# Second layer's first product by Strassen's scheme: seven block products, in three tiles of 768 tokens

## The chip, the cores and the metric

One program runs on one core of a Trainium2 chip. A core has TensorE (PE, matrix products, with its weight loads shown as PEld), VectorE (DVE), ScalarE (ACT), GpSimd (POOL) and SyncE (SP, which here only starts transfers). Each works through its own list of instructions in order, and they wait for each other by semaphores. The metric is the device time of one execution in microseconds (us); lower is better.

## The reference, cut to what matters

```
attn_out = softmax attention over means of 4 tokens, repeated 4 times
           + softmax attention within +-3 tokens          # 4 x 8 heads x 576 tokens x 64
x = attn_out as [2304, 512]
h = x @ w_in;   x = (s * relu(h)**2 + b) @ w_out          # 512 -> 2048 -> 512, first layer
h = x @ w_in2;  g = h - tanh(h);  out = g @ w_out2        # 512 -> 2048 -> 512, second layer
```

All values are float32. The change is in the last line alone.

## The kernel before, in words

**Numbers in two parts.** TensorE is fed with the type fp32r. Each operand a is kept as a "high" part (ACT copies a into an fp32r tile) and a "low" part (DVE or POOL subtracts the high part from a). A product is three matmuls that add up in PSUM: high by high, low by high, high by low.

**Stages.** Attention comes first, on all engines. The first layer runs over eight tiles of 288 tokens, and beside it runs the attention of the tokens to come. Its result goes turned, channels first, through the DRAM tensor x2T (ystage to x2T, `store1`), and the second layer loads it from there (`load_x2`).

**Second layer.** Six tiles of 384 tokens (`N2 = 384`, `TILES2 = 6`). Each tile has 16 turns f, one for 128 of the 2048 inner channels. A turn is:

- `hidden2` (L1922 to L1939): 12 matmuls (4 parts of the 512 channels, 3 products of parts), 384 columns each, into one of the two PSUM banks of `hid`.
- `tanh` (ACT, L1638), `difference` (DVE, `gdif`, L1361), `g2_high` (ACT, L1646), `g2_low` (DVE, L1370), one after the other, on 128 x 384 values.
- `output2` (L1941 to L1957), three turns later: 9 matmuls of 512 columns (3 groups of 128 tokens, 3 products of parts) that add into three banks of `acc` over the whole tile. In the last tile the last two turns of it are `last2` (L1967).

**Weights and tokens of the second layer.** The two weight matrices are loaded 1 MB at a time during the last tile of the first layer into the places of the first layer's weights (L938, L950) as soon as these are used up, and split once, 512 columns per instruction (`w2_high` on ACT, L1621, `w2_low` on DVE, L1343). They stay for all six tiles. The tokens of a tile are loaded (`load_x2`, L965) and split (`x2_split_high` on ACT, L1630, `x2_split_low` on DVE, L1351) a tile ahead, in two buffers. POOL has no work in the second layer.

**Order.** `plan()` lists all steps with an estimated cost, what they come after, and a rank; `Plan.run` places them one by one, the one that can start earliest first and the lower rank among equals, and so writes the order of each engine's list. The order is fixed when the program is built. It knows no interruption of an instruction and no effect of one engine on another's speed.

**First layer, where it touches the change.** POOL makes the low part of each turn's activations (`g_low`, `gl`, L1057, 128 x 288) between ACT's work and the `output1` of three turns later.

Of the kernel before, what the change touches and what calls it, by code (L numbers as in the profile page):

```python
# [49 lines left out]
N2 = 384  # L50
TILES2 = TOKENS // N2
LAG2, GRING2 = 3, 4
# [43 lines left out]
def turn_of(f, half):  # L96

    return f + LAG1 * half

# [131 lines left out]
def plan():  # L231
# [189 lines left out]
    for kind, turn in turns(TILES1, LAG1):  # L421
# [30 lines left out]
    for g in range(FT // WGROUP):  # L452
        for kind, user in (("load_w2a", "hidden1"), ("load_w2b", "output1")):
            o.add("SP", 0.6, (3, g), (kind, g), [(user, last, WGROUP * (g + 1) - 1)], kbytes=1024)
    for f in range(FT):
        for half in range(2):
            o.add("ACT", act(512), (2, f), ("w2_high", f, half), [(("load_w2a", "load_w2b")[half], f // WGROUP)])
            o.add("DVE", dve(512), (2, f), ("w2_low", f, half), [("w2_high", f, half)])
    for j in range(TILES2):
        after = [("x2_split_low", j - 1)] if j else [("add_up", SUBS - 1, NPART - 1)]  # L460
        o.add("SP", 0.6, (3, j), ("load_x2", j), after + [("store1", last_tile(j))], kbytes=800)
        o.add("ACT", KT * act(N2), (0,), ("x2_split_high", j),
              [("load_x2", j)] + ([("hidden2", j - 2, FT - 1)] if j > 1 else []))
        o.add("DVE", KT * dve(N2), (0,), ("x2_split_low", j), [("x2_split_high", j)])
    for kind, turn in turns(TILES2, LAG2):
        j, f = divmod(turn, FT)
        if kind == "hidden":
            after = [chain] + ([("w2_low", f, 0)] if j == 0 else [])
            after += [("x2_split_low", j)] if f == 0 else []
            after += [("difference", *divmod(turn - 2, FT))] if turn > 1 else []  # L470
            o.add("PE", 12 * mm(N2), (1,), ("hidden2", j, f), after)
            chain = ("hidden2", j, f)
            o.add("ACT", act(N2), (0,), ("tanh", j, f),
                  [chain] + ([("difference", *divmod(turn - 2, FT))] if turn > 1 else []))
            o.add("DVE", dve(N2), (0,), ("difference", j, f), [("tanh", j, f)])
            o.add("ACT", act(N2), (0,), ("g2_high", j, f), [("difference", j, f)] + (
                [("output2", *divmod(turn - GRING2, FT))] if turn >= GRING2 else []))
            o.add("DVE", dve(N2), (0,), ("g2_low", j, f), [("g2_high", j, f)])
        else:
            after = [chain, ("g2_low", j, f)] + ([("w2_low", f, 1)] if j == 0 else [])  # L480
            if f == 0:
                after += [("finish2", j - 1, i) for i in range(N2 // P)] if j else [("finish1", last)]
            if j == TILES2 - 1 and f >= FT - 2:

                if f == FT - 1:
                    for i in range(N2 // P):
                        o.add("PE", 6 * mm(DM), (1,), ("last2", i), after + [("g2_low", j, f - 1)])
                        after = [("last2", i)]
                    for i in range(2):
                        o.add(("DVE", "ACT")[i], 0.7, (0,), ("finish2", j, i), [("last2", i)])  # L490
                        o.add("SP", 1.2, (0, j, i), ("store_out", j, i), [("finish2", j, i)], kbytes=256)
                    for e in ("DVE", "ACT"):
                        o.add(e, 0.7, (0,), ("finish_last", e), [("last2", 2)])
                    o.add("SP", 0.6, (0, j, 2), ("store_out", j, 2), [("finish_last", "DVE")], kbytes=128)
                continue
            o.add("PE", 9 * mm(DM), (1,), ("output2", j, f), after)
            chain = ("output2", j, f)
            if f == FT - 1:
                for i in range(N2 // P):
                    o.add(("DVE", "ACT", "DVE")[i], 0.7, (0,), ("finish2", j, i), [chain])  # L500
                    if i != 1:
                        o.add("SP", 1.2, (0, j, i), ("store_out", j, i), [("finish2", j, i)], kbytes=256)
# [17 lines left out]
def build(nc, q, k, v, moe_w_in, moe_w_out, moe_s, moe_b, moe2_w_in, moe2_w_out, out):  # L520
# [104 lines left out]
    at[0] = o_att  # L625
    x2h, _ = place("x2h", [P, 2, KT, N2], F32R)
    x2l, _ = place("x2l", [P, 2, KT, N2], F32R)
    x2raw, _ = place("x2raw", [P, KT, N2], F32)
    tanh, _ = place("tanh", [P, 2, N2], F32)
    gdif, _ = place("gdif", [P, 2, N2], F32)  # L630
    ostage, _ = place("ostage", [P, 3, DM], F32)

    g2h, _ = place("g2h", [P, GRING2, N2], F32R, o_x)
    g2l, _ = place("g2l", [P, GRING2, N2], F32R, o_xh)
    assert GRING2 * N2 <= XRING * KT * NS
# [17 lines left out]
    s_x2raw = sem("s_x2raw")  # L653

# [12 lines left out]
    s_w2high, s_w2low = sem("s_w2high"), sem("s_w2low")  # L667
# [14 lines left out]
    s_x2h, s_x2l, s_h2, s_tanh = sem("s_x2h"), sem("s_x2l"), sem("s_h2"), sem("s_tanh")  # L682
    s_dif, s_g2h, s_g2l, s_used2 = sem("s_dif"), sem("s_g2h"), sem("s_g2l"), sem("s_used2")
    s_o = [sem(f"s_o{i}") for i in range(3)]
    s_last, s_oh = sem("s_last"), sem("s_oh")
    s_out = [sem(f"s_out{i}") for i in range(3)]
# [77 lines left out]
    def half_of(f, half, a, b):  # L764
        return a[:, :, f * P:(f + 1) * P] if half == 0 else b[:, f, :]
# [63 lines left out]

    def rows_of(j, i):  # L830
# [13 lines left out]
    def stored_count(j, i):  # L844

        return sum(len(rows_of(one, i)) for one in range(j + 1))

    def store_rows(e, j, i):
        for rows, row, pattern in rows_of(j, i):
            e.dma_start(dram(out, row * DM, pattern), ostage[rows, i, :]).then_inc(s_out[i], 16)  # L850

    def store_half(e, half):

        rows, row, pattern = rows_of(TILES2 - 1, 2)[half]
        e.dma_start(dram(out, row * DM, pattern), ostage[rows, 2, :]).then_inc(s_out[2], 16)
# [206 lines left out]
    def vector_program(ve):  # L1062
# [9 lines left out]
        for kind, *key in o.order["DVE"]:  # L1072
# [929 lines left out]
```

## Time and profile before

| | us |
|---|---|
| median of 3 runs | 911.38 |
| lowest and highest run | 910.88, 911.38 |
| span of the profiled execution | 909.3 |
| PE busy in it | 895.9 (99%) |
| DVE, ACT, POOL busy | 501.7, 425.0, 279.4 |
| chain that ended last: PE, ACT, DMA, DVE | 95%, 2%, 1%, 1% |

The span reaches from the first to the last instruction of the profiled execution. The profiled execution is given by its span alone; the median of the runs is 2.1 us above it, which is what lies around the span. The page's 40 slices of 22.7 us show PE at 9 tenths or more from the second to the 39th. The granted TensorE clock shows 9 (90% or more) in all of them, and its mean over the span is 0.998. From the 24th slice on DVE and ACT are busy two or three tenths, and POOL not at all: that is the second layer. A matmul's busy time is more than the time until the next one starts, since matmuls overlap; the time between starts is read from the chain or the timeline.

### The profile page before, as it was taken

Reading aid. Unit: us, or ns where it says so; the run is one execution under the profiler, and the core shown is the slowest. Engines: PE = TensorE matmul, PEld = TensorE weight load, DVE = VectorE, ACT = ScalarE, POOL = GpSimd, SP = SyncE. Lnnn points to the kernel's source line nnn. Section 1 sums busy time; section 2 is a strip of 40 time slices with the busy share of each in tenths; the row PEclk is TensorE's granted clock in tenths of the full one; section 3 lists DMA queues with packets and bytes.
Section 4 is the critical chain, followed back from the end, with each engine's and each line's share of the span. In section 5 each row is a group of like instructions: output and inputs, shape, how many; then the busy total and the mean of one; then the engine's idle time right before and its main releaser. Section 6 shows DMA issues by size and latency. Waiting matters only on the chain.

```text
span 909.3 us, 15682 instructions
## 1 busy us (share of the span) xinstructions
PE 895.9 (99%) x6100; PEld 846.0 (93%) x6100; DVE 501.7 (55%) x635; ACT 425.0 (47%) x1060; POOL 279.4 (31%) x280
## 2 busy tenths in 40 slices
PE   6999999999999999999999999999999999999998
PEld 6789999999999999999999999999999999999997
DVE  5658599989999999982104632323323323322322
ACT  2899585566546754446457722322323223222221
POOL 6568474966497653534222000000000000000000
PEclk9999999999999999999999999999999999999999
DMA  8962453343344223002225400200200100100101
GB/s 217 274 236 55 127 146 85 91 121 85 97 114 115 62 61 78 19 2 65 66 77 181 165 1 1 70 1 1 70 1 22 49 1 1 35 1 1 35 1 35
DMA packets 48333, 65.15 MB, mean 72 GB/s; under 512 B 18246, under 2 KB 30084, under 8 KB 48260
## 3 DMA queue, kind: packets, MB, share of 16 engines
q1 hardware_dynamic: 45865, 62.42, 24.8%
q10 hardware_dynamic: 2395, 1.74, 0.8%
q8 instruction: 48, 0.79, 0.4%
q14 instruction: 25, 0.20, 0.1%
HBM read 54.71 MB, written 9.44 MB: 71 GB/s over the span
## 4 chain that ended last, share of the span: by engine, by line
PE 95%; ACT 2%; DMA 1%; DVE 1%; issue 1%; SPq 1%; ACTq 0%; DVEq 0%
PE acc L1918 22%; PE hid L1937 22%; PE hid L1890 21%; PE acc L1955 21%; PE pa L1848 1%; PE pa L1815 1%; DMA dkey<-in_k_dram 1%; PE pa L1832 1%; PE pa L1690 1%; PE pa L1861 1%; PE acc L1967 0%; PE hid L1898 0%; SPq L867 0%; PE hid L1796 0%; PE pa L1753 0%
## 5 line engine op out<-in xcount | busy, mean ns | idle before, releaser
L1057 POOL TENSOR_TENSOR gl<-relu,gh 128x288 fp32r<-128x288 f32 x128 | 128.6, 1008 | 185.9 <-PE acc L1918 129.5
L1361 DVE TENSOR_TENSOR gdif<-hid,tanh 128x384 f32<-128x384 f32 x96 | 53.5, 558 | 184.4 <-ACT tanh L1638 184.2
L1918 PE MATMUL acc<-gh,wbh 128*128 128x288 f32 (+1 forms) x512 | 154.6, 302 | 0.0
L1890 PE MATMUL hid<-xh,wah 128*128 128x288 f32 x512 | 153.5, 301 | 0.3 <-ACT relu L1597 0.2
L1918 PE MATMUL acc<-gl,wbh 128*128 128x288 f32 (+1 forms) x512 | 151.5, 296 | 0.0
L1918 PE MATMUL acc<-gh,wbl 128*128 128x288 f32 (+1 forms) x512 | 151.1, 295 | 0.0
L1890 PE MATMUL hid<-xh,wal 128*128 128x288 f32 x512 | 150.4, 295 | 0.0
L1890 PE MATMUL hid<-xl,wah 128*128 128x288 f32 x484 | 142.0, 294 | 0.0
L1638 ACT ACTIVATE tanh<-hid 128x384 f32<-128x384 f32 x96 | 47.2, 491 | 186.3 <-PE hid L1937 186.3
L1937 PE MATMUL hid<-x2h,wal 128*128 128x384 f32 x384 | 129.0, 336 | 0.0
L1937 PE MATMUL hid<-x2h,wah 128*128 128x384 f32 x384 | 128.9, 336 | 0.0
L1937 PE MATMUL hid<-x2l,wah 128*128 128x384 f32 x384 | 128.8, 336 | 0.0
L1597 ACT ACTIVATE relu<-hid 128x288 f32<-128x288 f32 x128 | 52.3, 409 | 134.0 <-PE hid L1890 110.7
L1955 PE MATMUL acc<-wbl,g2h 128*128 128x512 f32 x282 | 110.2, 391 | 0.0
L1955 PE MATMUL acc<-wbh,g2l 128*128 128x512 f32 x282 | 110.0, 390 | 0.0
L1955 PE MATMUL acc<-wbh,g2h 128*128 128x512 f32 x282 | 109.9, 390 | 0.0
L1918 PEld LDWEIGHTS acc<-gh,wbh 128*128 128x128 f32 x512 | 96.5, 189 | 1.0 <-issue 0.4
L1890 PEld LDWEIGHTS hid<-xh,wah 128*128 128x128 f32 x512 | 96.2, 188 | 1.0 <-issue 0.6
L1918 PEld LDWEIGHTS acc<-gh,wbl 128*128 128x128 f32 x512 | 96.5, 188 | 0.0
L1918 PEld LDWEIGHTS acc<-gl,wbh 128*128 128x128 f32 x512 | 96.4, 188 | 0.0
L1890 PEld LDWEIGHTS hid<-xh,wal 128*128 128x128 f32 x512 | 96.3, 188 | 0.1
L1890 PEld LDWEIGHTS hid<-xl,wah 128*128 128x128 f32 x484 | 90.8, 188 | 0.0
(162 smaller groups left out, 1549.9 us busy)
## 6 DMA issues: line engine op xcount, KB each, us to landing
wa_raw<-in_moe_w_in_dram SPq DMA_DIRECT2D x8, 1024.0 KB, 7.8
wb_raw<-in_moe_w_out_dram SPq DMA_DIRECT2D x8, 1024.0 KB, 6.3
kl<-in_k_dram SPq DMA_DIRECT2D x23, 240.0 KB
vl<-in_v_dram SPq DMA_DIRECT2D x23, 240.0 KB
x2T<-ystage SPq DMA_DIRECT2D x8, 576.0 KB, 3.2
x2raw<-x2T SPq DMA_DIRECT2D x6, 768.0 KB, 4.5
own<-in_q_dram SPq DMA_DIRECT2D x11, 384.0 KB
ql<-in_q_dram SPq DMA_DIRECT2D x24, 144.0 KB, 2.9
```

The source lines that it names most:

```text
L1057: g.tensor_tensor(out=gl[:, turn % LRING1, 0:NS], in0=relu[:, f % 2, :], in1=gh[:, turn % GRING1, 0:NS].bitcast(F32), op=ALU.subtract).the ...
L1361: ve.tensor_tensor(gdif[:, f % 2, :], hid[:, f % 2, 0:N2], tanh[:, f % 2, :], ALU.subtract).then_inc(s_dif, 1)
L1597: sc.activation(r, hid[:, f % 2, 0:n], ACT.Relu).then_inc(s_relu, 1)
L1638: sc.activation(tanh[:, f % 2, :], hid[:, f % 2, 0:N2], ACT.Tanh).then_inc(s_tanh, 1)
L1690: one = pe.transpose(pa[0:HD, r, g * P:(g + 1) * P], src[:, g0 + g, :], ident[:, :])
L1815: one = pe.matmul(pa[0:2 * TQ, r, x * GROUPS:(x + 1) * GROUPS], apart[:, hp, x, :, :].rearrange("p t n -> p (t n)"), plain[:, hp, :], star ...
L1832: one = pe.transpose(pa[0:HG, r, x * 2 * TQ:(x + 1) * 2 * TQ], pc[0:2 * TQ, ones.start + x, kh * HG:(kh + 1) * HG], ident[0:2 * TQ, 0:2 * TQ])
L1848: one = pe.matmul(pa[h2 * HD:(h2 + 1) * HD, r, 0:cols.stop - cols.start], vd[0:HG, kh, 2 * hp + h2, :], pT[0:HG, h2, kh, cols], start=kh = ...
L1890: one = pe.matmul(dst, w[:, d, cols], x[:, j % XRING, d, :], start=i == 0, stop=i == 3 * KT - 1)
L1918: one = pe.matmul(acc[:, d, n], w[:, f, cols], g[:, turn % ring, n], start=(f == 0 and p == 0), stop=(f == FT - 1 and p == 2))
L1937: one = pe.matmul(hid[:, f % 2, 0:N2], w[:, d, f * P:(f + 1) * P], x[:, j % 2, d, :], start=(d == 0 and p == 0), stop=(d == KT - 1 and p = ...
L1955: one = pe.matmul(acc[:, i, :], g[:, f % GRING2, i * P:(i + 1) * P], w[:, f, :], start=(f == 0 and p == 0), stop=(f == FT - 1 and p == 2))
```

## The change

The first product of the second layer (x @ w_in2) is no longer 16 turns of 12 matmuls per tile. The token tile becomes 768 wide, three tiles. The 512 input channels are halved (A/B index 1 and 2), the 768 tokens of a tile are halved, and the inner channels are taken in pairs of 128. For each such pair ("quad" q, 8 per tile, block n = 8j + q) the 2 x 2 by 2 x 2 block product is made with seven products in place of eight (Winograd's form of Strassen's scheme). A product has 6 matmuls of 384 columns: two parts of 128 channels (kk) and the three products of parts.

```
S1 = A21+A22, S2 = S1-A11, S3 = A11-A21, S4 = A12-S2        (weights)
T1 = B12-B11, T3 = B22-B12, T2 = T3+B11, T4 = B21-T2        (tokens)
```

What is new in each place:

- PE, per block: `p1 p6 out p2 p7 out p4 p5 out p3 out out out`, where the six `out2` are those of the block before (6 matmuls of 512 columns each, six groups of 128 tokens, in four banks of `acc` and two of `pa`). All seven products share the two banks of `hid`: p1 then p2 on top of it and later p5, p3 on top of it, in bank 0; p6, then p7, p4 on top of it, in bank 1. Between them DVE and ACT take values out: p2 waits for `copy1` (ACT copies p1), p7 for `u2`, p4 for `u3`, p5 for the first difference, p3 for `c22`, the next p1 for `c12`.
- DVE, per block: five sums with a PSUM operand (u2, u3, c21, c22, c12), four differences, four `g2_low`, all 128 x 384. ACT, per block: `copy1`, four `tanh`, four `g2_high`.
- Weights of the first product: for each of the 8 quads four loads of 128 KB, four sums on DVE (`w2_sums`, 256 columns), one high part on ACT and one low part on POOL, each over 7 x 2 x 128 = 1792 columns in one instruction. Quads 0 and 1 can be loaded after turn 7 of the last tile of layer one, 2 and 3 after its last hidden turn, 4 to 7 after its last output. They stay for all three tiles.
- Weights of the second product no longer stay: for each of the 24 blocks 512 KB are loaded into a ring of two (`load_w2b`) and split by two ACT and two POOL instructions of 512 columns.
- Tokens: per tile seven blocks for each of two kk. POOL makes the four sums T1, T3, T2, T4 and the low parts of T3 and T4, ACT all high parts, DVE the other low parts. There is one buffer in place of two: a block's high part waits for the tile's last product that uses it (`XORDER` follows the order of the products).
- Block 0 takes the last three `output1` of the first layer as its only `out`.
- Results leave through three stages of 512 columns, of which two also hold T1 of the next tile.

```diff
-N2 = 384
+N2 = 768
 TILES2 = TOKENS // N2
-LAG2, GRING2 = 3, 4
+HALF2 = N2 // 2
+QUADS = FT // 2
+BLOCK2 = N2 // P
+PRODUCTS = {"p1": (A11, B11, 0, True), "p6": (S2, T2, 1, True), "p2": (A12, B21, 0, False),
+            "p7": (S3, T3, 1, True), "p4": (A22, T4, 1, False), "p5": (S1, T1, 0, True), "p3": (S4, B22, 0, False)}
+XORDER = (B11, T2, B21, T3, T4, T1, B22)
+POOL_LOWS = (T3, T4)
...
+        order = ["p1", "p6", outs[0], "p2", "p7", outs[1], "p4", "p5", outs[2], "p3"] + outs[3:]
...
+            elif kind == "w2a_low":
+                q, = key
+                g.wait_ge(s_w2ah, q + 1)
+                g.tensor_tensor(out=wql[q][:, :, :, :], in0=wq_raw[q][:, :, :, :], in1=wqh[q][:, :, :, :].bitcast(F32),
+                                op=ALU.subtract).then_inc(s_w2al, 1)
...
+            elif kind == "w2_sums":
+                q, = key
+                raw, a21 = wq_raw[q], wq_a21[q][:, :, :]
+                ve.wait_ge((s_wa + s_wb)[q], 16 + 64)
+                ve.tensor_tensor(raw[:, S1, :, :], a21, raw[:, A22, :, :], ALU.add).then_inc(s_w2sum, 1)
+                ve.tensor_tensor(raw[:, S3, :, :], raw[:, A11, :, :], a21, ALU.subtract).then_inc(s_w2sum, 1)
...
+            elif kind == "u3":
+                n, = key
+                if n:
+                    ve.wait_ge(s_g2l, 4 * (n - 1) + 3)
+                ve.wait_ge(s_u2, n + 1)
+                ve.wait_ge(s_product["p7"], n + 1)
+                ve.tensor_tensor(sum22[:, :], hid[:, 1, 0:HALF2], sum12[n % 2][:, :], ALU.add).then_inc(s_u3, 1)
...
+            elif kind == "product":
+                n, name = key
+                j, q = divmod(n, QUADS)
+                w, x, r, fresh = PRODUCTS[name]
+                if j == 0:
+                    pe.wait_ge(s_w2al, q + 1)
+                if q == 0:
+                    for kk in range(2):
+                        wait_low2(pe, j, kk, x)
...
+                for kk in range(2):
+                    for p, (wt, xt) in enumerate(((wqh[q], x2h), (wqh[q], x2l), (wql[q], x2h))):
+                        one = pe.matmul(hid[:, r, 0:HALF2], wt[:, w, kk, :], xt[:, x, kk, :],
+                                        start=fresh and kk == 0 and p == 0, stop=kk == 1 and p == 2,
+                                        skip_group_check=not fresh)
+                one.then_inc(s_product[name], 1)
...
+            elif kind == "out2":
+                n, i = key
+                j, q = divmod(n, QUADS)
+                if n == 0:
                     pe.wait_ge(s_y, KT * TILES1)
+                elif q == 0:
+                    pe.wait_ge(s_o[i], j)
+                pe.wait_ge(s_w2bl, 2 * (n + 1))
+                pe.wait_ge(s_g2l, 4 * n + (2 if i < BLOCK2 // 2 else 4))
```

## Rows read from the trace of the kernel before

**Rows 1.** The page: span, and busy us (share) xinstructions of each engine.
```profile
span 909.3 us, 15682 instructions
PE 895.9 (99%) x6100; PEld 846.0 (93%) x6100; DVE 501.7 (55%) x635; ACT 425.0 (47%) x1060; POOL 279.4 (31%) x280
```

**Rows 2.** Windows: length, busy us (xcount) of PE, PEld, DVE, ACT, POOL; clock, DMA, GB/s.
```profile
500.00:520.00 20.00, 20.00 (x130) 19.64 (x129) 11.44 (x21) 15.04 (x32) 1.61 (x2) 1.00 0.54 188
600.00:700.00 100.00, 100.00 (x509) 91.16 (x508) 30.39 (x55) 27.82 (x56) 0.00 (x0) 1.00 0.06 17
```

**Rows 3.** The chain of waits: start us, length us, what ran.
```profile
502.30 6.35 PE acc L1918 x48
508.65 8.32 PE hid L1937 x48
...
574.83 4.09 PE acc L1955 x18
578.92 4.16 PE hid L1937 x24
...
901.26 4.09 PE acc L1967 x18
...
905.44 0.68 DVE ostage L1386
```

**Rows 4.** Groups by shape: operation, tiles, shapes xcount | busy us, mean ns | idle before.
```profile
L1937 PE MATMUL hid<-x2h,wal 128*128 128x384 f32 x384 | 129.0, 336 | 0.0
L1638 ACT ACTIVATE tanh<-hid 128x384 f32<-128x384 f32 x96 | 47.2, 491 | 186.3 <-PE hid L1937 186.3
L1361 DVE TENSOR_TENSOR gdif<-hid,tanh 128x384 f32<-128x384 f32 x96 | 53.5, 558 | 184.4 <-ACT tanh L1638 184.2
L1646 ACT ACTIVATE g2h<-gdif 128x384 fp32r<-128x384 f32 x96 | 50.4, 525 | 67.9 <-DVE gdif L1361 67.9
L1351 DVE TENSOR_TENSOR x2l<-x2raw,x2h 128x384 fp32r<-128x384 f32 x24 | 12.7, 590 | 25.1 <-ACT x2h L1630 25.1
L1621 ACT ACTIVATE wah<-wa_raw 128x512 fp32r<-128x512 f32 x16 | 9.9, 619 | 0.0
```

**Rows 5.** Timeline near the end: start us, us, engine, line, operation [idle before <-releaser].
```profile
892.87 0.39 PE L1955 MATMUL acc<-wbh,g2h 128*128 128x512 f32 x1
893.13 0.49 ACT L1638 ACTIVATE tanh<-hid 128x384 f32<-128x384 f32 x1 [2.33 <-PE hid L1937]
893.75 0.56 DVE L1361 TENSOR_TENSOR gdif<-hid,tanh 128x384 f32<-128x384 f32 x1 [2.30 <-ACT tanh L1638]
894.40 0.53 ACT L1646 ACTIVATE g2h<-gdif 128x384 fp32r<-128x384 f32 x1 [0.78 <-DVE gdif L1361]
```

**Rows 6.** Timeline in the attention: POOL, DVE, and a PE step that waits for DVE.
```profile
32.57 1.28 POOL L1040 TENSOR_TENSOR wal<-wa_raw,wah 128x512 fp32r<-128x512 f32 x1
32.82 1.39 DVE L1110 TENSOR_TENSOR dprob<-dprob,dinv 128x330 f32<-128x330 f32 x1
34.26 0.25 PEld L1780 LDWEIGHTS acc<-ident,dprob 128*66 128x66 f32 x3 [0.83 <-DVE dprob L1110]
```

**Rows 7.** Timelines of POOL and DVE side by side, at three places.
```profile
77.06 1.55 POOL L1040 TENSOR_TENSOR wal<-wa_raw,wah 128x512 fp32r<-128x512 f32 x1
77.39 1.78 DVE L1178 TENSOR_TENSOR wal<-wa_raw,wah 128x512 fp32r<-128x512 f32 x1
...
157.55 3.27 POOL L1031 TENSOR_TENSOR own<-own 128x384 f32<-128x384 f32 x1
159.86 1.17 DVE L1336 TENSOR_TENSOR xraw<-pa,up 128x256 f32<-128x256 f32 x2
...
497.60 0.82 POOL L1057 TENSOR_TENSOR gl<-relu,gh 128x288 fp32r<-128x288 f32 x1 [2.38 <-PE acc L1918]
498.00 0.96 DVE L1343 TENSOR_TENSOR wal<-wa_raw,wah 128x512 fp32r<-128x512 f32 x1 [1.03 <-ACT wah L1621]
498.89 0.68 DVE L1343 TENSOR_TENSOR wbl<-wb_raw,wbh 128x512 fp32r<-128x512 f32 x1
```

**Rows 8.** Transfers: tiles, queue xcount, KB each, median us to landing.
```profile
x2T<-ystage SPq DMA_DIRECT2D x8, 576.0 KB, 3.2
wa_raw<-in_moe_w_in_dram SPq DMA_DIRECT2D x8, 1024.0 KB, 7.8
```

More of the change, by code:

```diff
@@ L420, in plan @@
                 o.add("POOL", 1.15, (0,), ("x_low", j, d), [("x_high", j, d)])
-    for kind, turn in turns(TILES1, LAG1):
+    for kind, turn in turns(TILES1, LAG1)[:-LAG1]:
         j, f = divmod(turn, FT)
@@ L451, in plan @@
     last = TILES1 - 1
[L452 to L458, printed above, removed]
-    for j in range(TILES2):
[L460 to L491, printed above, removed]
-                    for e in ("DVE", "ACT"):
[L493 to L502, printed above, removed]
@@ new lines, in plan @@
+    for q in range(QUADS):
+        after = [("hidden1", last, 7)] if q < 2 else [("hidden1", last, FT - 1)] if q < 4 else [("output1", last, FT - 1)]
+        if q == QUADS - 1:
+            after.append(("store1", last))
+        o.add("SP", 2.4, (3, 2 * q), ("load_w2a", q), after, kbytes=512)
+        o.add("DVE", 1.8, (2, q), ("w2_sums", q), [("load_w2a", q)])
+        o.add("ACT", 1.65, (2, q), ("w2a_high", q), [("w2_sums", q)])
+        o.add("POOL", 4.7, (2, q), ("w2a_low", q), [("w2a_high", q)])
@@ L622, in build @@
     lpT = behind("lpT", [P, BLOCKS, P], *room_band)
[L625 to L635, printed above, removed]
+    unit, quad = 4 * HALF2, 4 * 2 * 7 * 2 * P
@@ new lines, in build @@
+    o_ring = o_wbh
+    o_quads = [o_wah, o_wal, o_wah + quad, o_wal + quad] + [o_ring + 4 * 8 * DM + quad * i for i in range(3)]
+    o_g2 = o_x
+    o_quads.append(o_g2 + 4 * 4 * 4 * HALF2 * 2 // 2)
+    o_x2 = o_quads[-1] + quad
+    o_inter = o_x2 + 4 * 2 * 7 * 2 * HALF2
+    o_raw0 = o_inter + 5 * unit
+    o_raw1 = o_quads[6] + quad
+    assert o_raw1 + 4 * unit <= o_x and o_raw0 + 4 * unit <= nc.sbuf_usable_end and o_x2 >= o_att
+    wqh = [place(f"wqh{i}", [P, 7, 2, P], F32R, o_quads[i])[0] for i in range(QUADS)]
@@ new lines, in build @@
+    tanh11, _ = place("tanh11", [P, HALF2], F32, o_inter + 3 * unit)
+    tanh, _ = place("tanh", [P, HALF2], F32, o_inter + 4 * unit)
+    odd12, _ = place("odd12", [P, HALF2], F32, o_wal + 2 * quad + 4 * DM)
+    sum12 = (even12, odd12)
+    ostage = [place(f"ostage{i}", [P, DM], F32, o)[0]
+              for i, o in enumerate((o_wah + 2 * quad, o_wah + 2 * quad + 4 * DM, o_wal + 2 * quad))]
+    assert o_wal + 2 * quad + 4 * DM + unit <= o_wbh and o_wah + 2 * quad + 8 * DM <= o_wal
+    raw0, _ = place("x2raw0", [P, 2, N2], F32, o_raw0)
@@ L1889, in tensor_program @@
                             pe.wait_ge(s_x0l, d + 1)
-                    one = pe.matmul(dst, w[:, d, cols], x[:, j % XRING, d, :], start=i == 0, stop=i == 3 * KT - 1)
+                    one = pe.matmul(dst, w[:, group, d, cols], x[:, j % XRING, d, :], start=i == 0, stop=i == 3 * KT - 1)
                 if f or not j:
```

540 lines of the change are left out of this document (382 added, 158 removed).

## The prediction

> **What bounds the kernel now.** The page comes first: PE is busy 895.9 of 909.3 us, no other engine over 55% [rows 1]. A busy share says nothing yet of who is waited for, so the windows by stage are next: in the second layer PE is busy without a gap, 100.00 of 100.00 us, at full granted clock, DVE 30.4, ACT 27.8, POOL 0.0 [rows 2]. The chain of waits then shows that the end hangs on PE: from 508.65 us on, over the whole listing, `hidden2` and `output2` alternate with nothing between, to `last2` at 901.26, and only the last eviction follows, at 905.44 [rows 3]. From the chain come the times per matmul, too: 24 of `hidden2` in 4.16 us and 48 in 8.32, so 0.1733 us each; 18 of `output2` in 4.09, so 0.227 each. (The mean of 336 ns in the groups [rows 4] is the time in flight, not the pitch.) 1152 x 0.1733 + 864 x 0.227 = 199.7 + 196.1 = 395.8 us, and the chain has 905.35 - 508.65 = 396.7. The second layer is as long as its matmuls. So fewer matmuls pay in full, as long as the other engines, now less than a third busy, keep up.
>
> **What is removed.** Per tile of 768 and pair of 128 channels, the old form takes 2 x 4 x 3 matmuls for each half of the tokens, 48; seven products of six are 42. Over 24 blocks that is 1008 for 1152, all of the same 384 columns: 144 x 0.1733 = **-25.0 us**. `output2` keeps its 24 x 36 = 864. I take no price for changing groups more often: between the last `hidden2` matmul and the next step PE goes on at its pitch, though the new group has waits of its own [rows 5]. Bounds: 0 to 0.05 us (the time from a DVE end to PE's weight load, below) for each of the 312 groups less the 192 before, at most 6 us.
>
> **A block without disturbance.** A product takes 6 x 0.1733 = 1.04 us, an `out` 6 x 0.227 = 1.36, a block 7 x 1.04 + 6 x 1.36 = 15.45. Latencies from rows: PE to ACT 0.26 after the start of the next group (892.87 to 893.13), ACT to DVE 0.13, DVE to ACT 0.09 [rows 5], DVE to PE 0.05 (32.82 + 1.39 = 34.21 to 34.26) [rows 6]. The tightest waits are p4 on `u3` and p3 on `c22`, each with one `out` as its cover: 0.26 + 0.56 + 0.05 = 0.87 of 1.36, so DVE may be 0.49 late, some 0.27 if the weight load is to keep its lead of one matmul. Before `u3` stands the first difference: p2's end + 0.26 + 0.49 + 0.13 = 0.88, then 0.56, so DVE is free at 1.44, when `u3` could have begun at 1.04 + 0.26 = 1.30. It is 0.14 late, within the slack. p2 and p7 have cover of 2.4, the next p1 of 4.1. DVE's 13 operations of 0.56 are 7.3 us of 15.45, ACT's nine of 0.5 and two of 0.62 are 5.7. So an undisturbed block costs nothing. I take 1.5 us for all of them (bounds 0 and 24 x 2 x 0.3 = 14, if every such wait is 0.3 late). The tail is as before, six matmuls per group and halves at the end: 0.
>
> **The seam between the layers.** Block 0 has only three `out`. So p3 is followed at once by the next p1, which waits for c12: 0.26 + 0.56 + 0.05 = 0.87, and a weight load of 0.2: **+1.1 us**. Bounds 0.9 and 4 (if `finish1` on ACT is late too).
>
> **What POOL's new work does to DVE.** This is the large unknown. In the second layer POOL was idle; now it has 8 instructions of 1792 columns (`w2a_low`), 48 of 512 and 36 of 384. Its durations alone: 0.82 for 288 columns, 1.28 for 512 [rows 6, 7], 2.05 ns per column more, so 1.02 for 384 and **3.9 us for 1792**. The rows show what such an instruction does to DVE. POOL runs 77.06 to 78.61; a DVE subtraction of 512 columns with both operands in SBUF begins at 77.39 and takes 1.78, where it takes 0.68 alone (498.89): it ends 0.56 after POOL, as if it had stood still until then. Likewise 0.96 at 498.00 under a POOL instruction that ends at 498.42. But at 159.86 two DVE sums with one operand in PSUM take 1.17 together, inside a POOL instruction of 3.27 [rows 7]. So the five sums and the first difference of a block are free of it, and seven operations of a block (three differences, four `g2_low`), the 32 weight sums and the low parts of the tokens can each be held up for as long as one POOL instruction. DVE's list is in order, so `u3` and `c22` behind a held one are late as well.
>
> Only blocks of tile 0 meet the long ones. Quads 0 and 1 are made under the first layer, where a turn takes 24 x 0.132 = 3.2 us (6.35 us for 48 matmuls [rows 3]), POOL works 0.82 of it, and `output1` wants its result three turns, 9.5 us, after `hidden1`. One long instruction in front of it is covered: 0, or 2 x 1 us if two meet. Quads 2 to 7 come while blocks 0 to 3 run: 6 x 3.9 = 23 us of POOL. I place one such instruction at any point of a block. In the first four us after the block's last `g2_low` it holds nothing up; before the first `g2_low` it makes c22 up to 2.0 late (mean 0.5); later it makes c12 or the next u2 up to 2.3 late (mean 0.3 to 1.4). The mean over the block is 0.5 us. Where the four sums of the next quad (256 columns, 0.44 each by 0.56 for 384 and 0.68 for 512) are held in front of `u3` or `c22`, the lateness is up to 3.9 + 1.7 - 0.3, and its mean some 2.5. The quads' loads come close together, so I count four of the six at 2.0 and two at 0.5: **+9 us**. ACT's high part of 1792 columns (0.525 for 384 and 0.619 for 512 [rows 4], so 1.6) can make a `tanh` late too; that lies within these. Bounds: 0 (every one falls in a free place) and 23 (each is added in full).
>
> The Trainium skill says the same more sharply than the rows, which show no POOL instruction of 3.9 us without contention: "SBUF — State Buffer", section "Who interferes with whom", has a DVE instruction with two SBUF inputs and a GpSimd one that reads SBUF exclude each other, the first one holding the ports for its whole instruction. By it the upper bound of 23 us is possible; if a long instruction gave way between, the term would be near 1.
>
> **Changes of tile.** Twice, DVE gets 10 low parts of 0.59, ACT 14 high parts and half of six evictions, POOL some eight sums and low parts of 1.02 that hold DVE as above. They have two blocks (30.9 us) from the last p1 of a tile. DVE then has 2 x 7.3 + 5.9 + 2.0 = 22.5 us of work and perhaps 4 of holding, so no bound by throughput, but an operation of 0.6 in front of `u3` or `c22`, or one POOL instruction of 1.02, exceeds the 0.27 to 0.49. Ten such meetings of 0.25 us: **+5 us** for both. Bounds 0 and 16 x 1.02 = 16.
>
> Transfers: 512 KB per block against a median of 3.2 us for 576 KB [rows 8]. Landing 3.3 us after the block's start, ACT 1.2 and POOL 2.6 later, they are ready at 7.1, and wanted 17.5 us after that start. 0, with POOL's work beside them. These POOL instructions of 1.28 fall between 4 and 7 us of a block, mostly before its first `g2_low` at 6.6.
>
> **The sum.** -25.0 + 1.1 + 9 + 5 + 1.5 = -8.4. Made against the profiled span of 909.3 it gives 900.9; with the 2.1 us that the median of 911.38 lies above that span, **903 us**.
>
> **Rivals.**
> *Everything stays covered.* For it: DVE less than half busy, waits with slack in an undisturbed block, the order's own ranks. Against it: the held DVE operations of rows 7. -25.0 + 1.1 + 0.5: 888 us. Chance 0.22.
> *POOL and DVE exclude each other so much that it is slower.* Place: blocks 0 to 3. In about 60 us POOL's 23 + 10 (four blocks of `w2b_low`) + 4 (token sums) and DVE's 28 x 0.56 + 24 x 0.44 = 26 want the same thing, 63 us in all. Then PE waits nearly as long as POOL's long instructions last. It decides from the point where the held time exceeds the saved 25. -25.0 + 1.1 + 23 + 10 (tile changes at twice my term) + 2 = +11: 922 us. Against it: POOL and DVE also wait for loads and for ACT, which leaves gaps, and PE has 1.4 to 4 us of cover at most points. Chance 0.2.
> *The short covers fail in every block.* p4 and p3 each 0.3 late: 48 x 0.3 = 14.4, on top of 1.1 and 5, with the weights at 1: -3.5, 908 us. Against it the 0.49 worked out above. Chance 0.08.
> *The likeliest*, chance 0.5: 895 to 911.
>
> **How the numbers follow.** A measurement of this kernel tells 0.2%, 1.8 us, from no change. Faster: all of the first rival, 0.45 of the likeliest, 0.05 of the third, 0.72 together. Slower: the second rival, 0.20. Within 0.2%: the rest, 0.08. The range is to hold 8 in 10: from the covered case, 889 with a little loss, to 916, inside the slower case.
>
> **What would show it.** 42 matmuls on PE per block at 0.173, and a clean block of 15.45 us. PE's idle time should be put down to DVE, at p4 (u3), p3 (c22) and p1 (c12), and lie in the first four blocks and around the two changes of tile. There DVE operations with two SBUF operands should last 1 to 4.5 us in place of 0.56, each beginning under a POOL instruction, while u3 and c22 stay at 0.56. `w2a_low` should take 3.9 us. I am wrong if the clean blocks are longer than 15.6 us, if the pitch rises above 0.174, if the first layer's last tile gets longer, or if DVE is not held by the long instructions.

## The result, and the profile after

| | before | after |
|---|---|---|
| median of nine runs, us | 911.19 | 913.32 |
| lowest and highest | 909.78, 912.35 | 911.63, 914.59 |
| ratio, 95% interval | | 1.0028 [1.0018, 1.0038] |
| span of the profiled execution, us | 909.3 | 909.8 |
| its own time, us | | 912.1 |
| mean granted clock in it | 0.998 | 0.990 |

The prediction was 903 us, 8.4 faster; the kernel became 2.1 us slower. (913.3 lies within the stated 889 to 916, but on the other side of 911.) The saved matmuls are really gone, yet the time is not. First the page of the changed kernel, which answers to [rows 1]: the span, the engines' busy time, and two rows of the 40 slices.

```profile
span 909.8 us, 15887 instructions
PE 881.7 (97%) x5956; PEld 825.6 (91%) x5956; DVE 586.3 (64%) x759; ACT 465.6 (51%) x1128; POOL 421.9 (46%) x372
PE   6999999999999999999999787999999999999998
...
PEclk9999999999999999999999989999999999999999
```

There are 144 matmuls fewer (5956 for 6100), and PE is busy 14.2 us less, at a span 0.5 longer. The slices say where to look: PE falls from 9 to 7 and 8 in the 23rd to 25th, just where the second layer begins, and the granted clock falls with it in the 24th. The windows, which answer to [rows 2] (length, busy us of PE, PEld, DVE, ACT, POOL, clock, DMA, GB/s), give the size:

```profile
500.00:520.00 20.00, 15.32 (x99) 14.58 (x97) 13.35 (x17) 7.62 (x12) 14.20 (x8) 0.99 0.28 80
520.00:545.00 25.00, 20.29 (x79) 17.82 (x80) 20.10 (x28) 10.30 (x15) 10.77 (x5) 0.80 0.39 118
545.00:572.00 27.00, 21.82 (x101) 19.06 (x102) 17.86 (x23) 9.86 (x19) 10.50 (x4) 0.94 0.12 39
600.00:700.00 100.00, 99.55 (x497) 88.96 (x496) 54.79 (x93) 43.40 (x87) 32.63 (x26) 1.00 0.23 69
```

From 600 on PE is nearly as dense as before. Between 500 and 572 it stands idle 4.7 + 4.7 + 5.2 = 14.6 us, and the clock means 0.80 and 0.94. The chain of waits, which answers to [rows 3], shows a block without disturbance (start, length, what ran):

```profile
567.83 2.10 PE hid L2234 x12
569.93 1.39 PE acc L2251 x6
571.32 2.08 PE hid L2234 x12
573.40 1.39 PE acc L2251 x6
...
580.70 2.73 PE pa L2251 x12
583.43 2.10 PE hid L2234 x12
```

Twelve matmuls, of two products, in 2.08 are 0.1733 each, as before, and from 567.83 to 583.43 a block takes 15.60; over all matmul starts it is 15.61. Laying those starts out by block gives the account ("clean" is a block without disturbance, "over clean" what a block took beyond it):

```
block      0      1      2      3-6    7      8      9-14   15     16     17-22
took       18.08  24.27  22.77  15.61  15.75  16.61  15.61  15.71  16.57  15.61
over clean  5.98   8.66   7.16  0      0.14   1.00   0      0.10   0.96   0
(clean: 12.10 for block 0, whose only outs are the three output1 of 1.59 each; 15.61 for the others)
```

The last three `output1` of the first layer stand in block 0 now. With them counted in, the stretch to the end of the last matmul was 401.4 us before and is 403.2 now. Who holds PE up in the first three blocks is in the waits of PE (us in total, times, longest), from 502 to the end:

```profile
PE hid L2234 <- DVE sum L1613: 5.8, 3, 3.1
PE hid L2234 <- DVE even L1619: 4.1, 1, 4.1
PE acc L2251 <- DVE g2l L1633: 3.4, 1, 3.4
PE hid L2234 <- DVE odd L1619: 0.9, 1, 0.9
...
```

L1613 is `c22`, ahead of p3; L1619 is `c12`, ahead of the next p1; L1633 is `g2_low`, ahead of an `out2`. All three are DVE; the rest of the list is 1.1 us. But these are not slow operations themselves. Two timelines side by side, POOL first, then DVE (start, us, operation, idle before):

```profile
510.13 8.32 POOL L1241 TENSOR_TENSOR wql<-wq_raw,wqh 128x1792 fp32r<-128x1792 f32 x2 [2.89 <-ACT wqh L1883]
530.33 4.17 POOL L1241 TENSOR_TENSOR wql<-wq_raw,wqh 128x1792 fp32r<-128x1792 f32 x1 [11.89 <-ACT wqh L1883]
537.39 4.15 POOL L1241 TENSOR_TENSOR wql<-wq_raw,wqh 128x1792 fp32r<-128x1792 f32 x1 [2.88 <-ACT wqh L1883]
...
544.79 4.16 POOL L1241 TENSOR_TENSOR wql<-wq_raw,wqh 128x1792 fp32r<-128x1792 f32 x1 [0.93 <-ACT wqh L1883]
```

```profile
512.26 2.34 DVE L1633 TENSOR_TENSOR g2l<-tanh,g2h 128x384 fp32r<-128x384 f32 x1
514.52 0.55 DVE L1613 TENSOR_TENSOR sum<-hid,sum 128x384 f32<-128x384 f32 x1
514.99 3.87 DVE L1628 TENSOR_TENSOR sum<-sum,tanh 128x384 f32<-128x384 f32 x1
...
530.52 4.26 DVE L1574 TENSOR_TENSOR wq_raw<-wq_raw,wq_a 128x256 f32<-128x256 f32 x1
...
537.57 4.25 DVE L1576 TENSOR_TENSOR wq_raw<-wq_raw 128x256 f32<-128x256 f32 x1
...
545.00 4.23 DVE L1574 TENSOR_TENSOR wq_raw<-wq_raw,wq_a 128x256 f32<-128x256 f32 x1
```

Read the starts and ends together. The two POOL instructions of 510.13 end at about 514.3 and 518.45; the `g2_low` of 512.26 ends at 514.60, the difference of 514.99 at 518.86. A weight sum of 256 columns that begins 0.2 us after POOL (530.52 after 530.33) takes 4.26 in place of 0.42. The operation at 514.52 in between, `c22`, has an operand in PSUM and takes 0.55 beneath the second POOL instruction. The groups by shape say it for the whole layer (xcount, then busy us and mean ns):

```profile
L1628 DVE TENSOR_TENSOR sum<-sum,tanh 128x384 f32<-128x384 f32 x48 | 32.6, 680 | 1.5 <-ACT tanh L1922 1.5
L1633 DVE TENSOR_TENSOR g2l<-tanh,g2h 128x384 fp32r<-128x384 f32 x24 | 18.7, 781 | 11.5 <-ACT g2h L1929 11.5
L1613 DVE TENSOR_TENSOR sum<-hid,sum 128x384 f32<-128x384 f32 x24 | 13.3, 555 | 7.7 <-PE hid L2234 7.7
L1574 DVE TENSOR_TENSOR wq_raw<-wq_raw,wq_a 128x256 f32<-128x256 f32 x6 | 11.3, 1876 | 0.0
```

Same size, both operands in SBUF: 680 and 781 ns in the mean. One in PSUM: 555. The last row is the costliest: 1876 ns for an operation of 420. The held operations explain the waits in two ways. In block 0 it is a difference of the block itself, held at 514.99, that makes `c12` late, and PE waits 4.1 us. In block 2 a `g2_low` held at 557.62 (3.72 us, under POOL's instruction of 556.88) makes `c22` late by 1.8. And in blocks 1 and 2 the DVE list places the four sums of a later quad in front of `c22`, `c12` or a `g2_low` of the running block, POOL holds one of them for four us (530.52, 537.57, 545.00), and what PE waits for stands behind it, by 3.1, 0.9 and 3.4 us.

The second toll is TensorE's clock. The timeline of PE around 520, matmuls of the same shape (the one at 515.63 is from before the wait):

```profile
515.63 0.34 PE L2234 MATMUL hid<-x2h,wql 128*128 128x384 f32 x1
...
520.62 0.66 PE L2234 MATMUL hid<-x2h,wqh 128*128 128x384 f32 x1 [4.11 <-DVE even L1619]
521.08 0.52 PE L2234 MATMUL hid<-x2l,wqh 128*128 128x384 f32 x1
521.40 0.52 PE L2234 MATMUL hid<-x2h,wql 128*128 128x384 f32 x1
```

After 4.11 us of idling the pitch is 0.32 in place of 0.173. The granted clock stands at half, 1.2 GHz, from 519.69 for 6.83 us, from 536.76 for 3.41 and from 550.41 for 3.41. Each of these begins in the last microsecond of a wait of PE of 3.1 to 4.1 us. Windows laid inside the three stretches (13.4 us in all) show PE busy for 12.0, so up to half of that, 6 us, is the clock's toll (an estimate).

### The profile page after: what moved, and what is told of

Read it like the earlier page. It is cut to its first block, busy times and chain, and to the rows that moved or that the text cites. A ratio compares the mean times of both kernels' runs of the same rounds, so it can differ in the third digit from the quotient of the medians.

```text
span 909.8 us, 15887 instructions
## 1 busy us (share of the span) xinstructions
PE 881.7 (97%) x5956; PEld 825.6 (91%) x5956; DVE 586.3 (64%) x759; ACT 465.6 (51%) x1128; POOL 421.9 (46%) x372
## 4 chain that ended last, share of the span: by engine, by line
PE 88%; DVE 7%; ACT 2%; issue 2%; DMA 1%; SPq 1%; ACTq 0%; DVEq 0%
PE acc L2197 22%; PE hid L2169 21%; PE hid L2234 18%; PE acc L2251 13%; PE pa L2251 6%; DVE wq_raw L1574 1%; PE pa L2127 1%; PE pa L2094 1%; DVE sum L1628 1%; DMA dkey<-in_k_dram 1%; PE pa L2111 1%; PE pa L1969 1%; DVE x2l L1583 1%; DVE g2l L1633 1%; PE pa L2140 1%
## 5 line engine op out<-in xcount | busy, mean ns | idle before, releaser
L1233 POOL TENSOR_TENSOR gl<-relu,gh 128x288 fp32r<-128x288 f32 x128 | 131.4, 1031 | 150.1 <-PE acc L2197 106.6
L1249 POOL TENSOR_TENSOR w2bl<-w2b_raw,w2bh 128x512 fp32r<-128x512 f32 x48 | 63.3, 1339 | 211.1 <-ACT w2bh L1890 211.1
L2234 PE MATMUL hid<-x2h,wqh 128*128 128x384 f32 x336 | 115.0, 342 | 12.0 <-DVE sum L1613 5.8
L2234 PE MATMUL hid<-x2l,wqh 128*128 128x384 f32 x336 | 114.0, 339 | 0.0
L2234 PE MATMUL hid<-x2h,wql 128*128 128x384 f32 x336 | 113.7, 338 | 0.0
L2234 PEld LDWEIGHTS hid<-x2h,wqh 128*128 128x128 f32 x336 | 64.0, 190 | 19.9 <-issue 13.6
L2251 PE MATMUL acc<-w2bh,g2h 128*128 128x512 f32 x192 | 75.9, 396 | 3.4 <-DVE g2l L1633 3.4
L2251 PE MATMUL acc<-w2bh,g2l 128*128 128x512 f32 x192 | 77.0, 401 | 0.0
L2251 PE MATMUL acc<-w2bl,g2h 128*128 128x512 f32 x192 | 76.8, 400 | 0.0
```

Of the source, the lines that this page charges most:

```text
L1233: g.tensor_tensor(out=gl[:, turn % LRING1, 0:NS], in0=relu[:, f % 2, :], in1=gh[:, turn % GRING1, 0:NS].bitcast(F32), op=ALU.subtract).the ...
L1249: g.tensor_tensor(out=w2bl[:, slot, :], in0=w2b_raw[:, slot, :], in1=w2bh[:, slot, :].bitcast(F32), op=ALU.subtract).then_inc(s_w2bl, 1)
L2234: one = pe.matmul(hid[:, r, 0:HALF2], wt[:, w, kk, :], xt[:, x, kk, :], start=fresh and kk == 0 and p == 0, stop=kk == 1 and p == 2, skip_ ...
L2251: one = pe.matmul(out_bank(i), g[:, n % 2, f, i * P:(i + 1) * P], w[:, slot, :], start=(q == 0 and f == 0 and p == 0), stop=(q == QUADS - ...
```

## The experiments

Two theories at the start. A: a POOL instruction holds a DVE operation with two SBUF operands until it ends, so the length of `w2a_low` is what costs. B: the DVE list itself is the fault, four weight sums in one step ahead of what PE waits for. The medians of before beside these runs were 911.19 (first four), 911.22 (next four) and 910.88 (last two); each ratio is against these. In experiments 1, 2, 5 and 6 the time came out 0.2 to 2.3 us below what A had foretold, in 3 it came out 0.8 above.

**1. `w2a_low` in seven instructions of 256 columns**, order and data as they were; PE's wait counts seven pieces per quad.

```diff
-                g.tensor_tensor(out=wql[q][:, :, :, :], ...)
+                for one in range(7):
+                    g.tensor_tensor(out=wql[q][:, one, :, :], ...)
```

> The changed kernel with one edit: POOL makes the low part of a quad's weights in seven instructions of 256 columns instead of one of 1792; order of every list unchanged. Theory A (a POOL instruction shuts out DVE operations with two SBUF operands for its whole length; six long ones cost the new kernel most of the 22 us that blocks 0 to 2 take beyond 12.1, 15.6 and 15.6): no DVE operation is held longer than some 0.8 us, the three blocks take 8 to 12 us beyond the clean length instead of 22, the clock falls less often, time 900 to 904. Theory B (the order is at fault: weight sums stand in DVE's list ahead of u2 and u3; the holding is incidental): the same 1792 columns on POOL, same order, so within 2 us of the changed kernel, 911 to 914.

Measured: 897.74 us, ratio 0.9852 [0.9837, 0.9867]. Blocks 0 to 2 took 14.17, 17.24 and 18.51. The timeline, POOL first and then DVE:

```profile
525.81 12.67 POOL L1242 TENSOR_TENSOR wql<-wq_raw,wqh 128x256 fp32r<-128x256 f32 x14 [3.22 <-ACT wqh L1884]
```

```profile
530.52 0.96 DVE L1577 TENSOR_TENSOR wq_raw<-wq_raw 128x256 f32<-128x256 f32 x1
531.51 0.85 DVE L1579 TENSOR_TENSOR wq_raw<-wq_raw 128x256 f32<-128x256 f32 x1
532.28 1.09 DVE L1629 TENSOR_TENSOR sum<-sum,tanh 128x384 f32<-128x384 f32 x1
533.30 0.55 DVE L1620 TENSOR_TENSOR odd<-hid,odd 128x384 f32<-128x384 f32 x1
```

POOL works longer now, 12.67 for two quads where two whole instructions took 8.32, and DVE is held at every turn, but for one piece each, 0.5 us and not 4. The longest wait of PE was 1.3, and the clock did not fall in this layer. 15.6 us for a cut in one instruction: A holds. POOL's longer work is now itself waited for:

```profile
PE hid L2235 <- POOL wql L1242: 2.4, 3, 1.3
```

**2. The whole `w2a_low`, but later**: those of quads 2 to 7 wait, in the plan and on POOL, for the last `g2_low` of the block two before.

```diff
+                if q > 1:
+                    g.wait_ge(s_g2l, 4 * (q - 2) + 4)
                 g.wait_ge(s_w2ah, q + 1)
```

> The changed kernel with the 1792-column instructions of quads 2 to 7 kept whole but each made to wait for the last g2_low of the block two before the one that uses it, so that one falls in each of blocks 1 to 6 at its start, where DVE has no operation with two SBUF operands for some 6 us. Theory A (place of the long POOL instructions): holds of 4 us vanish or fall where nothing waits; the loss over clean blocks falls from 22 us to 5 to 8, time 896 to 901. Theory B (weight sums ahead of u2, u3 in DVE's list; they are untouched here): loss stays at 12 or more, time 903 to 912. A third view, that the preparation work is simply too much for the engines: no change, 911 to 914.

Measured: 895.70, ratio 0.9824 [0.9808, 0.9841]. Blocks 13.57, 19.76, 15.63, then 15.61. The instructions are as long as ever; spread over the blocks and put where DVE has little of that kind they cost nothing, but for one in block 1 (POOL, then DVE):

```profile
522.67 4.07 POOL L1243 TENSOR_TENSOR wql<-wq_raw,wqh 128x1792 fp32r<-128x1792 f32 x1 [14.81 <-DVE g2l L1635]
```

```profile
523.60 3.42 DVE L1575 TENSOR_TENSOR wq_raw<-wq_a,wq_raw 128x256 f32<-128x256 f32 x1
```

That one made p3 2.3 us late, and the clock fell for 3.41 us behind it. The place counts as much as the length.

**3. The four weight sums as four steps of the plan**, so that urgent work can go between.

```diff
-        o.add("DVE", 1.8, (2, q), ("w2_sums", q), [("load_w2a", q)])
+        for m in range(4):
+            o.add("DVE", 0.43, (2, q), ("w2_sums", q, m), [("load_w2a", q)])
```

> The changed kernel with one edit: the four weight sums of a quad are four steps of the plan instead of one of 1.8 us, so that product steps of the same moment come between; POOL's 1792-column instructions unchanged. Theory A (holding by POOL): at most 3 us gained, 909 to 913, and DVE operations of 4 us still there. Theory B (order): most of the 22 us gained, 895 to 901.

Measured: 913.79, ratio 1.003 [1.002, 1.004], no better than the change itself. Blocks 19.26, 17.68, 29.07, with 20.48 us at half clock. The timeline, POOL and then DVE, shows why the finer order doesn't help: whichever operation with two SBUF operands comes next is caught.

```profile
540.72 4.13 POOL L1242 TENSOR_TENSOR wql<-wq_raw,wqh 128x1792 fp32r<-128x1792 f32 x1 [3.43 <-ACT wqh L1890]
```

```profile
540.89 4.25 DVE L1580 TENSOR_TENSOR wq_raw<-wq_raw 128x256 f32<-128x256 f32 x1
```

B as the main cause falls. What the order costs can be read from block 0: 13.56 with the sums in one step (experiments 2 and 5), 13.04 with the sums apart (6 to 10), so 0.5 us.

**4. What the clock costs.** Twenty matmuls into a bank not in use fill the first long wait, ahead of p1 of block 1; they compute nothing that is used.

```diff
+                    if n == 1:
+                        for _ in range(20):
+                            pe.matmul(pa[:, 1, 0:HALF2], wqh[0][:, 0, 0, :], x2h[:, 0, 0, :], start=True, stop=True)
```

> The changed kernel with 20 more matmuls of 384 columns (3.5 us, results unused) in front of the p1 of block 1, where PE stood idle 4.4 us and after which its granted clock was 0.5 for 6.83 us. Theory C (the idle time takes a second toll through the clock, some 3 us here): block 1 runs its first groups at 1.04 and 1.39 instead of 2.06, 1.92 and 2.27, the first stretch at 0.5 is gone, and the kernel gains 2 to 4 us, 909 to 911. If the clock fell for another reason or the slow groups hid behind DVE anyway: no change or up to 1 us slower, 913 to 914.

Measured: 909.91, ratio 0.9990 [0.9981, 0.9999], 3.4 us below the change. The first stretch at half clock is gone (the next begins at 536.43), the first product of block 1 takes 1.16 for 2.06, and the block 21.59 for 24.27, 2.7 us less. The other two stretches stay. The toll is real; it is a part of what the waits cost, not a cause beside them.

**5. The most that `w2a_low` can cost.** Of quads 2 to 7 only 256 of the 1792 low columns are made, and PE multiplies by the low parts of quads 0 and 1.

```diff
+                some = slice(0, 7) if q < 2 else slice(0, 1)
...
-    ..., (wql[q], x2h))):
+    ..., (wql[q % 2], x2h))):
```

> The changed kernel without the long POOL work: of quads 2 to 7 only 256 of the 1792 columns of the low part are made, and TensorE reads the low parts of quads 0 and 1 in their place; same order of all lists, the eight-in-a-row weight sums and all ACT work kept. Theory A with its price: what is left beyond clean blocks (12.1 for block 0, 15.6 each for 1 and 2) is the seam of 1.1 us and the order's share, 3 to 5 us together, against 22 in the changed kernel and some 7 with seven short instructions: 893 to 897. Theory B (order) would leave 12 us or more: 904 or above.

Measured: 892.82, ratio 0.9800 [0.9784, 0.9815]. Blocks 13.56, 15.75, 15.80, then 15.61. So the long instructions of these six quads cost 913.3 - 892.8 = 20.5 us. (Six pieces of 256 columns, one per quad, are still made.)

**6. The same work on DVE.** `w2a_low` as seven DVE steps of 256 columns, the weight sums apart.

```diff
-        o.add("POOL", 4.7, (2, q), ("w2a_low", q), [("w2a_high", q)])
+        for m in range(7):
+            o.add("DVE", 0.43, (2, q), ("w2a_low", q, m), [("w2a_high", q)])
```

> The low parts of the quads' weights on DVE instead of POOL, as seven steps of 256 columns that the plan may place apart, the four sums apart too. DVE gets 6 x 7 x 0.34 = 14 us more within the first blocks, POOL's holding is gone. Theory A: worth it, 894 to 898, no operation of DVE over 1.3 us (the 512-column POOL instructions stay). Rival D (DVE itself is short of time in the first blocks, holding or not): 901 or more, with DVE busy over 9 tenths between 505 and 550 us.

Measured: 892.50, ratio 0.9797 [0.9782, 0.9813]: as good as leaving the work out. Windows of two of the first blocks:

```profile
517.00:532.00 15.00, 14.26 (x73) 12.97 (x73) 13.07 (x28) 7.39 (x14) 2.22 (x2) 1.00 0.76 232
532.00:548.00 16.00, 16.00 (x81) 14.15 (x80) 15.46 (x38) 10.67 (x16) 2.74 (x2) 1.00 0.11 34
```

In the second window DVE is busy 15.46 of 16 us, and PE 16.00. (In the first, PE's 0.7 us of idle time are the seam's wait for `c12`.) A full engine that is held for 1.5 us at most harms next to nothing here; one with less work of its own, held four us at a time, does.

**7. Gated lows, and the weight sums apart and gated too** (from quad 3 on, behind `copy1` of the block two before).

```diff
+                if q > 2:
+                    ve.wait_ge(s_copy1, q - 1)
```

> The gated long instructions, and beside it the four weight sums apart and those of quads 3 to 7 held until copy1 of the block two before the one that uses them, so preparation is one quad per block. In the gated kernel block 1 still lost 4 us because the sums of the next quad met the one long instruction and stood ahead of u3 and c22. Theory A: block 1 falls to 15.6 to 16.5, blocks 2 to 6 stay at 15.6, and the time is 891 to 894. If instead the order now puts a held sum ahead of u3 in each block: each of blocks 1 to 5 loses 1 to 2 us, 897 to 902.

Measured: 899.34, ratio 0.9875 [0.9859, 0.9890], 3.6 worse than experiment 2. Blocks 13.04, 16.54, 17.58, 17.15, 17.15, 17.12, 15.61. POOL, then DVE:

```profile
535.27 4.05 POOL L1244 TENSOR_TENSOR wql<-wq_raw,wqh 128x1792 fp32r<-128x1792 f32 x1 [2.12 <-DVE g2l L1644]
```

```profile
536.08 3.52 DVE L1579 TENSOR_TENSOR wq_raw<-wq_a,wq_raw 128x256 f32<-128x256 f32 x1 [0.89 <-ACT even L1918]
539.52 0.54 DVE L1602 TENSOR_TENSOR even<-hid,even 128x384 f32<-128x384 f32 x1
```

The gate let the first sum go just under the long instruction, ahead of `u2`, in each of four blocks. It is the second of the two cases in the expectation. What was free in experiment 2 costs 1.5 to 2.0 us per block: no rule of the kind "put it late" is safe while the instruction is long.

**8. The gates of 7 with the seven pieces of 1.**

> As the kernel with gated long instructions and gated sums, with the low part in seven instructions. Theory A: both cures act on the same loss, so nothing adds up; within 1 us of that kernel, 891 to 894, and the best of all so far by less than the noise. If the length of the holds mattered by itself even in the free part of a block: 1 us or more better.

Measured: 893.16, ratio 0.9807 [0.9790, 0.9825]; blocks 13.04, 15.69, 15.78, 15.61, 16.15, 15.62. The same gates at the same places, and the short pieces take 6.2 us off 7: again the second case, the length matters by itself.

**9. Fewer waits on PE** (from 6): `out2` waits only in the first and fourth of its six groups, where the others' waits are met already. Asked was where the 0.16 us of a clean block come from.

```diff
-                pe.wait_ge(s_w2bl, 2 * (n + 1))
-                pe.wait_ge(s_g2l, 4 * n + (2 if i < BLOCK2 // 2 else 4))
+                if i == 0:
+                    pe.wait_ge(s_w2bl, 2 * (n + 1))
+                if i % 3 == 0:
+                    pe.wait_ge(s_g2l, 4 * n + (2 if i < BLOCK2 // 2 else 4))
```

> The kernel with the low parts on DVE, and in each group of output matmuls only the waits that are not already covered by an earlier group of the same block (12 groups of 36 keep one). Question: why a clean block takes 15.61 us and not 7 x 1.04 + 6 x 1.363 = 15.45, some 3.7 us over 23 blocks. If the waits at the head of a group break TensorE's pace: 15.5 or less per clean block, 889 to 891. If it is the change of shape itself (384 columns to 512 after a product): 15.61 as before, 892 to 893.

Measured: 892.47, ratio 0.9798 [0.9782, 0.9815]. A clean block is still 15.61, and an `out` that lost its waits and follows a product still takes 1.39; the waits are not it. Blocks 2 and 3 took 16.81 here, for POOL's pair of 512 columns began 4.4 us after the start of block 2, where in 6 it was 5.5 (POOL, then DVE):

```profile
536.75 2.80 POOL L1246 TENSOR_TENSOR w2bl<-w2b_raw,w2bh 128x512 fp32r<-128x512 f32 x2 [6.01 <-ACT w2bh L1899]
```

```profile
536.87 1.52 DVE L1580 TENSOR_TENSOR wq_raw<-wq_raw 128x256 f32<-128x256 f32 x1
538.31 1.52 DVE L1571 TENSOR_TENSOR wq_raw<-wq_a,wq_raw 128x256 f32<-128x256 f32 x1
539.76 0.54 DVE L1608 TENSOR_TENSOR sum<-hid,even 128x384 f32<-128x384 f32 x1
```

**10. The low parts of T3 and T4 on DVE as well** (from 6).

```diff
-POOL_LOWS = (T3, T4)
+POOL_LOWS = ()
```

> The kernel with the low parts of the weights on DVE, and the low parts of the token blocks T3 and T4 on DVE as well, so that at a change of tile POOL only makes four sums per half. Question: where the 1.1 us of each change of tile come from. If from POOL holding DVE (Theory A, small instructions): 0.5 us or more less at each change, blocks 8 and 16 at 16.1 or less. If from ACT and DVE being given high and low parts ahead of copy1 and the last token part (order): no gain, or blocks 8 and 16 at 16.6 to 17.5 since DVE gets four operations more; 892 to 894.

Measured: 890.83 (889.18 to 892.55), ratio 0.9782 [0.9762, 0.9803]: the fastest, 20.1 us below before. Blocks 8 and 16, 16.61 and 16.57 after the change and 16.6 in experiments 1, 2, 3, 5 and 6, are 15.61. After the change PE had waited in each of the two for `copy1` on ACT (0.4 us, not the whole loss); in block 8 ACT was late because a difference that it needed took DVE 1.47 us (at 646.79) beneath POOL's low parts. The whole second layer has 0.9 us of waits of PE left:

```profile
PE hid L2243 <- DVE even L1628: 0.7, 1, 0.7
PE hid L2243 <- DVE tanh L1634: 0.2, 1, 0.2
```

## Why the prediction was wrong, step by step

| term | predicted | measured |
|---|---|---|
| fewer matmuls | -25.0 | pitch 0.1733 kept, 144 gone: -25.0 |
| undisturbed blocks | +1.5 | 23 x 0.16 = +3.7, or +2.8 beyond the kernel before, which took 0.9 more than its matmuls at pitch (396.7 for 395.8) |
| the seam | +1.1 | +0.9 (block 0 is 13.04 without other disturbance, for 12.10) |
| POOL's long instructions | +9 | 21.8 over clean in blocks 0 to 2, less the seam: +20.9 |
| changes of tile | +5 | 0.14 + 1.00 + 0.10 + 0.96 = +2.2 |
| sum | -8.4 | +2.7, and +1.8 when those 0.9 are taken off; the stretch itself grew by 1.8, the medians differ by 2.1 |

**The failed step** is "What POOL's new work does to DVE", and in it the size: +9 was put there, and it was +20.9. Of these, 0.9 stay when the long work is left out (experiment 5). Its mechanism was right in each point that the forecast named: operations of two SBUF operands lasting from 2.3 to 4.3 us, each begun under a POOL instruction, sums with a PSUM operand at 0.555 throughout, `w2a_low` of about 4.1 (3.9 was said). The Trainium skill, "SBUF — State Buffer", section "Who interferes with whom", says that a DVE instruction with at most one SBUF input, outside the 2-port modes, does not contend with GpSimd, and that one with two contends with a GpSimd instruction that reads SBUF; the trace agrees, with 0.55 at 514.52 and 3.87 at 514.99 beneath the same POOL instruction. My upper bound of 23, every long instruction in full, was nearly reached: 20.5 by experiment 5, 20.9 by the blocks. One place was not named in the forecast, the `out2` that waited 3.4 us for a `g2_low` behind a held weight sum (545.00).

Three things made 9 into 21. First, I placed a long instruction "at any point of a block" and averaged over a DVE that is mostly free. In these blocks it is not: DVE has its own seven such operations and the four sums of each coming quad, and most of the held ones begin 0.2 to 0.7 us after POOL (530.52, 537.57, 545.00, 514.99), so nearly the whole instruction is added. That DVE was busy 30% before [rows 2] said nothing of this stretch, where it is 20.10 of 25, held time included. Second, I counted each meeting by itself. Two long instructions came back to back at 510.13, before any block had given the slack back, and one held operation passes its delay to `c22`, `c12` and the `g2_low` behind it. Third, the granted clock. The forecast did not mention that it could fall. It did, for 13.65 us; experiment 4 took one of the three falls away and gained 3.4 in the median, 2.7 in the block itself.

**The rival that came true** was the second: POOL and DVE exclude each other in the first blocks. It put the held time at 23 us with 10 more from the tile changes and 2 beside, and said 922. In fact 20.9 for the long ones, 2.2 at the changes, 3.7 in the clean blocks and 0.9 at the seam came together: the limit of 25 was passed with the help of terms that I had thought small, and only just, 913. It deserved more than 0.2, since the holding on which it rests stood in the rows. Experiments 1, 5 and 6 agree that without the long instructions it is 892.5 to 897.7, near the "covered" rival's 888.

**Smaller steps.** The forecast said it would be wrong if clean blocks exceeded 15.6: they take 15.61. The six matmuls of an `out` that follows a product take 1.39 for 1.36, the first product of a block 1.07 for 1.04; this lies within the bound that was given for changes of group (at most 6), of which I took nothing. Waits are not its cause (experiment 9); what is stays open. The clean blocks have no wait of PE for `u3` or `c22`, so the rival of the short covers is refuted. Tile changes cost less than half of what was said, and experiment 10 shows that all of block 8's and 16's loss goes when the low parts leave POOL (eight of 1.41 us in the mean). The loads were no term, rightly: 512 KB landed in 3.5 us in the median, `w2b_low` took 1339 ns, and neither appears among PE's waits. (By holding DVE `w2b_low` can cost something, too: block 2 of experiment 9 took 16.81 for 15.61.)

```profile
L1249 POOL TENSOR_TENSOR w2bl<-w2b_raw,w2bh 128x512 fp32r<-128x512 f32 x48 | 63.3, 1339 | 211.1 <-ACT w2bh L1890 211.1
...
w2b_raw<-in_moe_w_out_dram SPq DMA_DIRECT2D x24, 512.0 KB, 3.5
```

**What is shown and what is argued.** Shown: that `w2a_low` on POOL in long instructions costs 20.5 us (5, 6), 15.6 of them by its length alone (1), that its place can avoid most of it (2) or not (7), that its pieces make the place indifferent (8), that the order of the sums alone does not (3), and the toll of one clock fall (4). Argued only: how the 20.9 divide between held time and clock beyond that one fall.

## What to carry to other kernels

Before work is given to an idle engine, ask what it locks while it works: POOL was free, but an instruction of it on SBUF stops the two-operand work of DVE until it ends. Keep such instructions short (seven pieces gave back 15.6 of 20.5 us, although POOL then worked half as long again), or give the work to the engine that would be held, even if that fills it to 97%. And where an average says "half a microsecond per meeting", look up how many meetings fall into the same slack of an in-order list, and whether PE would idle long enough to lose its clock on top.

## What the runs showed of the hardware beyond that

- PE pays twice for one wait. Its granted clock fell to half near the end of waits of 3.1 to 4.1 us in the changed kernel, and 0.8 us after the end of one of 2.3 in experiment 2 (3.41 us at half). After a wait of 1.8 in the changed kernel (ended at 562.42), and with waits of 1.3 and less (experiments 1, 7, 8, 10), it kept the full clock in the second layer.
- A POOL subtraction of 1792 columns takes 4.05 to 4.17 us and one of 512 1.34: 2.1 to 2.2 ns per column. It is hardly lengthened by DVE beside it, while DVE's operation lasts ten times as long (0.42 to 4.26). In pieces of 256 both sides lose: POOL takes 0.905 per piece in experiment 1, 6.3 per quad for 4.15, and DVE's sums 0.85 to 0.96 for 0.42.
- Where POOL's short instructions fall changes from one execution to another: nearly the same list of instructions gave blocks 2 and 3 of 15.83 and 15.70 in experiment 6 and 16.81 and 16.80 in 9, though the two differ only in waits on PE. Why the pair came earlier was not tried. One profile each can't explain a difference of 1 to 2 us between such kernels.
- Six matmuls of 512 columns behind a product take 1.39 us for 1.36, four times a block, and the first product of a block 1.07 for 1.04: 0.15 of the 0.16 us. The products after the other `out` groups lose nothing (2.08 for twelve matmuls). The change of width alone is not shown to be the cause: in the kernel before, nine matmuls of 512 behind twelve of 384 took 2.05 us for 2.04.
